# A gated linear attention kernel: wide matmuls for two levels, and five moves in the order of the start

## The reference

```python
f = 1.0 / (1.0 + np.exp(-f_logit))
for t in range(S):                     # gated linear attention, per batch and head
    state = f[:, :, t, :, None] * state + np.einsum('bhd,bhe->bhde', k[:, :, t], v[:, :, t])
    y[:, :, t] = np.einsum('bhd,bhde->bhe', q[:, :, t], state)
h = y.transpose(0, 2, 1) @ U @ V       # mixing over tokens, rank 32; y as batch x token x 384
u = y + h.transpose(0, 2, 1)
out1 = u + np.maximum(u @ w_ch1, 0.0) @ w_ch2
# gated FFN: h = relu(out1 @ w_in), a convolution of 3 taps over the tokens, gate = sigmoid
out = (h * gate) @ w_out
```

## Time and profile before

| | |
|---|---|
| median of 3 runs | 711.5 us (709.66 to 712.64) |
| profiled execution | 710.85 us, span 708.8 us |
| PE busy | 681.4 us, 96% of the span |
| weight loads busy | 644.6 us, 91% |
| VectorE, ScalarE, GpSimd busy | 441.1, 249.2, 264.2 us |
| chain that ended last | PE 92% |

### The profile page before, as it was taken

One profiled execution on the slowest core, in us unless ns is written; L12 is line 12 of the kernel. 1 busy time (PEld: TensorE's weight loads), 2 busy tenths in 40 slices (PEclk: granted clock), 3 DMA queues, 4 the chain that ended last, 5 costly groups with the idle time before them and its releaser, 6 DMA issues.

```text
span 708.8 us, 22548 instructions
## 1 busy us (share of the span) xinstructions
PE 681.4 (96%) x10084; PEld 644.6 (91%) x10084; DVE 441.1 (62%) x746; ACT 249.2 (35%) x509; POOL 264.2 (37%) x243
## 2 busy tenths in 40 slices
PE   3787899999999999999999999999999999999997
PEld 2786799999999999999999899999999999999997
DVE  6986776764887754464697855365498651222875
ACT  2044534252355413122246432213145541121553
POOL 5673465462542333162263324143253210030432
PEclk9999899999999999999999999999999999999999
DMA  8331544322002001201201110100000100000000
GB/s 196 107 93 42 132 124 134 104 80 68 2 25 80 34 25 24 68 4 45 48 2 57 47 58 15 55 25 25 25 1 2 36 35 1 1 0 1 1 35 33
DMA packets 22847, 33.46 MB, mean 47 GB/s; under 512 B 3712, under 2 KB 15744, under 8 KB 22752
## 3 DMA queue, kind: packets, MB, share of 16 engines
q1 hardware_dynamic: 21536, 30.07, 15.5%
q10 hardware_dynamic: 1216, 1.97, 1.1%
HBM read 27.31 MB, written 4.72 MB: 45 GB/s over the span
## 4 chain that ended last, share of the span: by engine, by line
PE 92%; DVE 2%; issue 2%; POOL 2%; DMA 1%; ACT 1%; SPq 0%; DVEq 0%; POOLq 0%
PE acc L806 8%; PE att L669 7%; PE acc L807 7%; PE acc L811 7%; PE hb L787 7%; PE hb L788 7%; PE hb L789 7%; PE acc L846 5%; PE hb L826 5%; PE hb L828 5%; PE acc L854 5%; PE hb L827 5%; PE acc L847 5%; PE att L715 3%; DMA k_t<-in_kT_dram 1%
## 5 line engine op out<-in xcount | busy, mean ns | idle before, releaser
L1236 DVE SCALAR_TENSOR_TENSOR r_lo<-hb,r_hi 128x386 fp32r<-128x386 f32 (+1 forms) x96 | 53.5, 557 | 176.1 <-ACT r_hi L982 176.1
L982 ACT ACTIVATE r_hi<-hb 128x386 fp32r<-128x386 f32 (+1 forms) x96 | 47.2, 492 | 247.6 <-PE hb L789 247.6
L1333 POOL TENSOR_TENSOR k_t<-k_t,blocks 112x512 f32<-112x512 f32 x60 | 80.8, 1349 | 137.3 <-PE att L669 130.7
L1372 POOL TENSOR_TENSOR r_lo<-conv,r_hi 128x384 fp32r<-128x384 f32 x64 | 63.6, 994 | 141.4 <-ACT r_hi L997 141.4
L806 PE MATMUL acc<-r_hi,w_ch_hi 128*128 128x386 f32 (+1 forms) x288 | 103.1, 358 | 0.0
L787 PE MATMUL hb<-u_hi,w_ch_hi 128*128 128x386 f32 (+1 forms) x288 | 97.8, 340 | 0.7 <-POOL w_ch_lo L1345 0.7
L788 PE MATMUL hb<-u_hi,w_ch_lo 128*128 128x386 f32 (+1 forms) x288 | 97.4, 338 | 0.0
L807 PE MATMUL acc<-r_hi,w_ch_lo 128*128 128x386 f32 (+1 forms) x288 | 97.3, 338 | 0.0
L789 PE MATMUL hb<-u_lo,w_ch_hi 128*128 128x386 f32 (+1 forms) x288 | 96.9, 337 | 0.0
L1266 DVE SCALAR_TENSOR_TENSOR conv<-hb,convw,conv 128x384 f32<-128x384 f32 x128 | 79.1, 618 | 4.5
L669 PEld LDWEIGHTS att<-q_t,k_t 48*64 48x64 f32 (+5 forms) x3840 | 59.2, 134 | 19.6 <-issue 16.8
(11 more groups left out here) (157 smaller groups left out, 1252.7 us busy)
## 6 DMA issues: line engine op xcount, KB each, us to landing
v_p<-in_vn_dram SPq DMA_DIRECT2D x12, 384.0 KB, 3.9
out_dram<-ostage SPq DMA_DIRECT2D x23, 192.0 KB, 2.1
gates<-in_fT_dram SPq DMA_DIRECT2D x20, 192.0 KB, 3.5
q_t<-in_qT_dram SPq DMA_DIRECT2D x20, 192.0 KB, 3.6
k_t<-in_kT_dram SPq DMA_DIRECT2D x20, 192.0 KB, 3.4
ostage<-in_w_ch_dram SPq DMA_DIRECT2D x14, 192.0 KB, 2.9
conv<-in_w_ch_dram SPq DMA_DIRECT2D x10, 192.0 KB, 2.7
ostage<-in_w_out_dram SPq DMA_DIRECT2D x5, 192.0 KB, 2.4
```

## The change

It has six parts.

1. The levels of 16 and 32 of duos 0 to 2 (`both_chunks`) take the keys of both chunks of a unit as weights, 112 or 96 columns, and move the odd blocks of the queries of both chunks, 64 columns. So there are 16 calls in place of 32, and the blocks between the two chunks are computed too and not read. ScalarE's copies have the same sizes and read the second chunk from columns 32 on.
2. `consts()` is issued by SP between the first and the second unit of duo 0.
3. Level 1 of duo 0 comes ahead of the gates and step EVEN of duo 1, on every engine (the key 0.6 for `(1, EVEN)`). The keys of the Y steps are as before.
4. `EARLY_K` = 3: duo 2's first key product is on VectorE too, and GpSimd's part of that step waits for its gates instead of q.
5. The three mix tasks come ahead of pieces 3 to 5.
6. The second batch's attention, duos 3 to 5, comes one slot later, on all engines, with its loads. Where slots are doubled, from 24 on, it comes two later.

```diff
-    steps = sorted((i + 1.5 * n + (1.25 if (n, st) == (0, Y) else 0.75 * (st == Y)), n, st)
+    later = {(0, Y): 1.25, (1, Y): 0.75, (2, Y): 0.75, (1, EVEN): 0.6}
+    steps = sorted((i + 1.5 * n + later.get((n, st), 0), n, st)
...
-            order += [("piece", FIRST + i) for i in range(3)] + [("mix", 0, i) for i in range(CT)] + [("level0", DUOS)]
+            order += [("mix", 0, i) for i in range(CT)] + [("piece", FIRST + i) for i in range(3)] + [("level0", DUOS)]
...
-                    s = (len(STEPS) + 1) * j + i + (st == Y and j < DUOS - 1) - (st == EVEN or (j, st) == (0, 0)) - (b == 0)
+                    s = (len(STEPS) + 1) * j + i + (st == Y and j < DUOS - 1) - (st == EVEN or (j, st) == (0, 0))
...
-EARLY_K = 2
+EARLY_K = 3
...
+        def both_chunks(n, st):
+            return n < DUOS and st >= LEVELS - 2
...
             for u in range(2):
+                if u == 1 and par == 0:
+                    consts()
...
+                    if both_chunks(n, st):
+                        for u in range(2):
+                            for r in range(PAIRS):
+                                for par in range(2):
+                                    rows, first, g = slice(C * par, C * par + D), at(u, r, 0), u * PAIRS + r
+                                    moving = split_blocks(q[rows, first:first + P], c)[:, :, 1, :]
+                                    mm = pe.matmul(banks[0:P - c, par, g * C:(g + 1) * C], k[rows, first:first + P - c],
+                                                   moving, start=True, stop=True, skip_group_check=True)
+                        mm.then_inc(level_done, 1)
+                        return
...
+                            first = c * pair + (C // 2 * half if both_chunks(n, st) else 0)
...
+                        first = C // 2 * half if both_chunks(n, st) else 0
```

More of the change, by code:

```diff
@@ L465, in weights_split, with consts @@
                 engine.wait_ge(w_lo_more, low_halves(n, True))
+        def consts():
+            nc.sync.dma_start(x[:, 0, 0:LEVELS * 32], mask_in).then_inc(loaded_masks, 16)
+            nc.sync.dma_start(x[:, 1, 0:P], ident_in).then_inc(loaded_masks, 16)
         def load_first(engine, par):
             for u in range(2):
+                if u == 1 and par == 0:
+                    consts()
                 done = [unit_f, unit_q, unit_k] if u == 0 else [loaded_f[0], loaded_q[0], loaded_k[0]]
@@ L539, in piece @@
                     loaded_w[i % STAGES], 16)
-            def consts():
-                sp.dma_start(x[:, 0, 0:LEVELS * 32], mask_in).then_inc(loaded_masks, 16)
-                sp.dma_start(x[:, 1, 0:P], ident_in).then_inc(loaded_masks, 16)
             def consts_mix():
@@ L562, in _ @@
                         load_first(sp, 0)
-                        consts()
                         continue
@@ L915, in attention @@
                             rows = slice(C * half + 2 * c * pair, C * half + 2 * c * pair + c)
+                            first = c * pair + (C // 2 * half if both_chunks(n, st) else 0)
                             nc.scalar.copy(
                                 scores[set_of(n)][rows, :].rearrange("p (g n c) -> p g n c", n=4, c=c)[:, :, 2 * pair + 1, :],
-                                banks.rearrange("p b (g x) -> p (b g) x", x=C)[rows, :, c * pair:c * pair + c]).then_inc(
+                                banks.rearrange("p b (g x) -> p (b g) x", x=C)[rows, :, first:first + c]).then_inc(
                                     quarters_taken, 1)
@@ L928, in attention @@
                         rows = slice(C * half, C * half + C // 2)
+                        first = C // 2 * half if both_chunks(n, st) else 0
                         nc.scalar.copy(
                             scores[set_of(n)][rows, :].rearrange("p (g two c) -> p g two c", two=2, c=C // 2)[:, :, 1, :],
-                            banks.rearrange("p b (g x) -> p (b g) x", x=C)[rows, :, 0:C // 2]).then_inc(last_taken, 1)
+                            banks.rearrange("p b (g x) -> p (b g) x", x=C)[rows, :, first:first + C // 2]).then_inc(last_taken, 1)
                 elif st == T:
```

## The result

The changed kernel takes 718.31 us in the median of 4 runs (717.91 to 719.58), the one before 711.73 us (709.66 to 712.64, 4 runs): a ratio of 1.0100, with a 95% interval from 1.0086 to 1.0114. The profiled executions have spans of 716.2 us and 708.8 us, 7.4 us apart. I forecast 716 us from a sum of +5.0 us. Of all the runs in this document one is left out of its median and ratio, since it stands far above the others of its kernel (729.36 us, of the wide levels with matmuls without a use throughout).

The account below looks back on a forecast made before the run. TensorE was taken as the bound behind 75 us; before 33.66 us VectorE and GpSimd. Terms -1.8 + 10.2 + 0.5 - 1.85 - 0.4 - 0.7 - 1.0 = +5.0 us gave 716 us, range 707.5 to 720.5.

Parts of the forecast that it names:

- The wide levels: Levels of 16 and 32 of three duos on TensorE: bursts cost their weight columns at 1.2 GHz, +10.2 us.
- Rival 1: Wide levels: loads of wide tiles are hidden and only the moving side counts; 710 us, chance 0.17.
- rival 4: Wide levels: the two halves of the array's rows do not overlap; 733 us, chance 0.05.
- Rival 2: TensorE's clock rises sooner, about 45 us instead of 57.6 us; -9.7 us, 707 us, chance 0.13.
- Change of tile: TensorE's 12 changes between 64 x 128 and 64 x 64 tiles: 0.04 us each, +0.5 us, bounds 0 and 3 us.
- Instruction supply: 384 fewer TensorE instructions: both "issue" waits before the output step go, -1.85 us; behind it -0.4 us.
- rival 3: Clock rises later, output steps and rank step at 1.2 GHz: +1 to +4, 718 to 720; 0.15 with rival 5.
- The front: Four edits up to duo 0's level of 16 at 33.66 us, -1.8 us: constants, level 1's order, third key product.
- third key product: Front: duo 2's key product moved to VectorE at 0.69 us; duo 0's level of 16 sooner, -2.2 us.
- rival 5: The front gives nothing, VectorE being the bound there: +2, 718 us; chance 0.15 together with rival 3.
- Mix: Behind 75 us, mix ahead of pieces 3 to 5: u_lo comes sooner, ending TensorE's wait at 78.58 us, -0.7 us.
- Slot: Second batch a slot on: TensorE's wait for VectorE at duo 3's level of 2, 87.38 us, is covered; -1.0 us.

Follow-up runs that it names:

- the kernel with 32 moving columns: Changed kernel's wide levels (112 or 96 weight columns), moving only the first chunk's queries, second chunk's scores left out; 720.12 us in its one run.
- part 1 alone: Kernel before with only the wide levels of 16 and 32 added; 718.48 us, ratio 1.0107.
- the five moves: Changed kernel with its levels of 16 and 32 narrow as before, so the other five parts only; 712.28 us, ratio 1.0015 to the kernel before.
- mix and slot: Kernel before with only mix tasks ahead of three pieces and the second batch a slot later; 709.94 us, ratio 0.9978.
- the order alone: Kernel before with only level 1 of duo 0 put ahead of duo 1's first step; 711.61 us, ratio 1.0005.
- the kernel with wide levels and fillers to 33 us: Wide levels plus matmuls without a use in TensorE's idle times up to 33 us; 720.43 us, ratio 1.0126 to the kernel before.
- fillers between the narrow levels: Kernel before, narrow levels, plus matmuls without a use up to 33 us and between the levels; 717.09 us, ratio 1.0087.
- the wide kernel: Wide levels of 16 and 32 plus matmuls without a use up to 33 us and between the levels; 712.97 us, ratio 1.0029 to the kernel before.

## Why the forecast came out as it did

**The wide levels: right.** +8.80 us against +8.85 us for the stretch. The burst of two costs what its weight columns say, 2 x 112 / 1.2 = 187 ns and an end, 3.25 us measured. Rival 1, only the moving side counts, is dead by this and by the kernel with 32 moving columns; rival 4, the row halves one after the other, is dead by the same 3.25 us, since it asked for twice as much. Rival 2, a rise of the clock about 45 us, did not come: the transposes at 66.92 us still take 1.76 us.

**Change of tile: right in size, its cause not shown.** Start to start the six wide levels take three times 3.18 and 2.75 us. The six narrow ones took 1.31, 1.44 and 1.39 us (levels of 16) and three times 1.01 us (levels of 32). That is 10.6 us more, where the terms gave 10.2 us. The rows of the kernel before that this needs beside the earlier trace rows:

```profile
34.97 1.91 PE L669 MATMUL hb<-q_t,k_t 48*62 48x32 f32 x64
...
50.60 1.46 PE L669 MATMUL hb<-q_t,k_t 48*48 48x32 f32 x64
51.99 1.75 PE L679 MATMUL acc<-ident_r,k_t 112*128 112x112 f32 x8
```

The +0.4 us left over stand against +0.5 us. No run has changes of tile alone, so they can also be ends of levels that overlap less.

**Instruction supply: right.** No "issue" wait is left between the level of 16 and the output step. The 10.6 us less the two waits of 1.86 us are 8.8 us, the 8.80 us measured. Behind it, from output step to rank step, the -0.53 us (-0.4 forecast) is right by luck, a net of two things of which the term held only one. The "issue" waits there were 0.7, 2.3 and 0.6 us before and one of 2.06 us after, 1.5 us less. The first output step now runs at 1.2 GHz, 1.95 and 1.96 us where it took 1.14 and 1.15 us, 1.6 us more; later steps give some of that back. So rival 3 came true for the first output step, though not for the rank step, and fewer waits hid its cost. How late the clock rises differs: with part 1 alone it was up at 66.41 us, where the same step takes 1.18 us.

**The front: this step failed.** It said -1.8 us and was +2.0 us. What failed in it first is the price of the third key product, -2.2 us. I priced it at the 0.69 us of the earlier trace rows and took GpSimd for the bound. In the run of this edit alone VectorE's products took 1.1 to 1.6 us, since each waited for GpSimd's, and VectorE was the bound: TensorE waits 1.88 us for its scores at 31.83 us. The level of 16 came 0.24 us sooner and the kernel was 0.16% slower. This is the condition of rival 5. Its 718 us is near the 718.3 us measured, but it took the front for nothing, where it cost 2.0 us. The constants were priced at -0.4 us; alone they moved nothing (+0.03 us). The exchange of order, +0.8 us, was -0.3 us. Each is one execution, within the spread given above.

These three add up to about -0.5 us, while the five moves together start the level at 34.58 us, +0.9 us. The times say the same: the ratios of the three alone add up to 1.0020, while the five moves (1.0015) against mix and slot (0.9978) leave 0.37%, an estimate of 2.6 us for the front as a whole. So more than 1 us comes from the edits meeting. My reading is that the delay of the keys is no longer covered once the order is exchanged. The traces fit: VectorE begins duo 1's first product at 18.63 us with the five moves and at 17.54 us with the order alone, 1.1 us apart. No pair of edits was run, so this is not shown. The remaining 1.1 us between the five moves' start and that of the changed kernel, whose front is the same, includes 0.8 us by which the keys arrived later in the one execution than in the other.

**Mix: right, with a gain beside it that was not forecast.** Timeline of PE in the changed kernel, against the earlier trace rows:

```profile
85.17 0.45 PE L789 MATMUL hb<-vstack,rstack 96*128 96x386 f32 x1 [0.39 <-DVE rstack L1235]
...
86.87 0.41 PE L804 MATMUL hb<-u_hi,w_ch_hi 128*128 128x386 f32 x1
```

From the first mix product to the first product pass 1.70 us, where it was 2.38 us (76.20 to 78.58): -0.7 us, as forecast. The other 1.3 us of the stretch's 1.97 us lie ahead of that, and are mainly the clock's. Before, TensorE was at 1.2 GHz again, as this row of the kernel before shows (columns as above), and the rank step took 2.78 us. After, it took 2.01 us and didn't fall again.

```profile
68.00:74.00 6.00, 5.40 (x76) 2.82 (x75) 1.22 (x3) 1.09 (x3) 3.45 (x4) 0.50 0.47 129
```

That second fall isn't in every execution. Of 29 of the kernel before on one chip, 6 had a mean clock of 0.998 or more, and their median was 709.2 us; the 23 others, at 0.992 to 0.995, had 711.9 us.

**Slot: right.** -0.89 us against -1.0 us, and the wait of the level of 2 is gone.

So the forecast stands on its largest term. The 3.8 us missed in the front were covered for a third by the clock behind it, which no step of mine had named. That part is luck: without it the spans would be 8.7 us apart, against 5.0 us forecast.

## What to carry to other kernels

Fewer matmuls are a gain only where their count, their supply or the moving side sets the pace. Two rows that differ in one size only (here 48 and 32 weight columns) tell which side that is, before anything is built. A product moved from GpSimd to VectorE must be priced as it runs beside GpSimd (1.61 us in the kernel before, not 0.69 us), and a load put ahead of others must be priced by what it delays, not by the wait that it ends.

## What the runs showed of the hardware that was not expected

- TensorE busy for 23.00 of 23 us with the steps of the attention stayed at 1.2 GHz (the kernel with wide levels and fillers to 33 us), and so it did for 16.00 of 16 us with fillers between the narrow levels. In the wide kernel the same fillers went with 1.00 from 33 to 60 us.
- The clock column showed 1.00 over stretches that ran at 1.2 GHz, up to the first change on record. The durations of equal instructions are the safer reading.
- A VectorE product of 0.69 us took up to 1.8 us where it began while a GpSimd instruction ran, and ended 0.55 to 0.64 us after that one. GpSimd's own took 1.5 to 1.9 us where VectorE's came between, and 1.15 us after its wait at 33.76 us.
- The "issue" waits of TensorE stood some 127 matmuls and as many weight loads apart, or multiples of that, and were 0.2 to 2.3 us long.
